# Twelve low-part splits moved behind the last gate, and eight raw loads moved one weight set later

## The reference, cut to what matters

```
attn_out = ...                         # decayed linear attention, 2 x 8 heads x 768 x 64
x = attn_out as 1536 tokens x 512
h = x @ w_in;  g = maximum(0.01 * h, h);  y = g @ w_out       # 512 -> 2048 -> 512
a = y @ w1;  b = y @ w2                                       # 512 -> 1024 each
out = ((a * b) @ w3) @ moe2_w_out                             # 1024 -> 1024 -> 512
```

## Time and profile before

| | us |
|---|---|
| median of 3 runs (519.84 to 519.9) | 519.85 |
| the profiled execution, its own time | 518.86 |
| its span, first to last instruction | 517.0 |
| TensorE busy in it | 507.7 |
| VectorE busy | 354.6 |
| ScalarE busy | 200.7 |

### The profile page before, as it was taken

How to read it: one execution, slowest core, us unless ns; L and a number is a source line. 1 busy time by engine, 2 the same in 40 slices (tenths; PEclk the granted TensorE clock), 3 DMA queues, 4 the chain that set the end, 5 groups by cost and what they waited for, 6 DMA issues and landing times.

```text
span 517.0 us, 9127 instructions
## 1 busy us (share of the span) xinstructions
PE 507.7 (98%) x3580; PEld 418.9 (81%) x3580; DVE 354.6 (69%) x539; ACT 200.7 (39%) x356; POOL 93.8 (18%) x101
## 2 busy tenths in 40 slices
PE   8999999999999999999999999999999999999796
PEld 6788888888888888888888888888888888888585
DVE  4757356767777876687755877697777754799732
ACT  5444253343456533233312455333333315475300
POOL 2223132112102321122200031122333100000000
PEclk9999999999999999999999999999999999999899
DMA  8998582433131111111100212111221107230102
GB/s 292 348 395 296 166 294 85 150 124 125 41 90 39 45 33 42 41 42 41 42 0 1 61 41 83 61 62 61 63 61 62 41 7 279 82 122 0 42 20 102
DMA packets 26666, 51.46 MB, mean 100 GB/s; under 512 B 3824, under 2 KB 4088, under 8 KB 26624
## 3 DMA queue, kind: packets, MB, share of 16 engines
q1 hardware_dynamic: 24144, 43.39, 25.3%
q10 hardware_dynamic: 2448, 7.49, 4.3%
q0 software_dynamic: 32, 0.00, 0.0%
HBM read 45.63 MB, written 5.25 MB: 98 GB/s over the span
## 4 chain that ended last, share of the span: by engine, by line
PE 87%; DVE 7%; DMA 2%; ACT 2%; issue 2%; SPq 1%; DVEq 0%; ACTq 0%
PE acc L1438 11%; PE acc L1439 11%; PE acc L1440 11%; PE hid L1650 10%; PE hid L1651 10%; PE hid L1649 10%; PE hid L1438 5%; PE hid L1440 4%; PE hid L1439 4%; DVE wa_lo L1040 2%; DMA stage<-weights 2%; PE hid L1470 1%; PE hid L1485 1%; PE acc L1777 1%; PE acc L1775 1%
## 5 line engine op out<-in xcount | busy, mean ns | idle before, releaser
L1438 PE MATMUL acc<-g_hi,wb 128*128 128x512 f32 x224 | 87.6, 391 | 0.0
L1440 PE MATMUL acc<-g_hi,wb 128*128 128x512 f32 x224 | 87.2, 389 | 0.0
L1439 PE MATMUL acc<-g_lo,wb 128*128 128x512 f32 x224 | 87.2, 389 | 0.0
L714 POOL TENSOR_TENSOR w_in_lo_place<-stage 128x256 f32<-128x256 f32 x16 | 12.8, 799 | 211.4 <-PE hid L1651 121.0
L1438 PE MATMUL hid<-xy_hi,wa_hi 128*128 128x512 f32 x128 | 50.2, 393 | 0.0
L1440 PE MATMUL hid<-xy_hi,wa_lo 128*128 128x512 f32 x128 | 49.8, 389 | 0.0
L1439 PE MATMUL hid<-xy_lo,wa_hi 128*128 128x512 f32 x128 | 49.8, 389 | 0.0
L1650 PE MATMUL hid<-wa_lo,wa_hi 128*128 128x512 f32 x128 | 49.8, 389 | 0.0
L1651 PE MATMUL hid<-wa_hi,wa_lo 128*128 128x512 f32 x128 | 49.8, 389 | 0.0
L1649 PE MATMUL hid<-wa_hi 128*128 128x512 f32 x128 | 49.8, 389 | 0.0
L1438 PEld LDWEIGHTS acc<-g_hi,wb 128*128 128x128 f32 x224 | 42.0, 188 | 8.9
(11 more groups left out here) (228 smaller groups left out, 935.7 us busy)
## 6 DMA issues: line engine op xcount, KB each, us to landing
stage<-weights SPq DMA_DIRECT2D x109, 256.0 KB, 3.4
w_out_place<-attn ACTq DMA_DIRECT2D x12, 512.0 KB, 5.7
x_hi_place<-attn SPq DMA_DIRECT2D x4, 512.0 KB, 8.5
w_out_place<-attn SPq DMA_DIRECT2D x4, 512.0 KB, 7.4
w_dram<-x_lo_place SPq DMA_DIRECT2D x8, 256.0 KB, 5.4
stage<-w_dram SPq DMA_DIRECT2D x8, 256.0 KB, 2.7
outT<-x_hi_place SPq DMA_DIRECT2D x7, 256.0 KB, 3.0
x_lo_place<-attn SPq DMA_DIRECT2D x2, 512.0 KB, 6.5
```

The source lines that it names most:

```text
L714: nc.gpsimd.tensor_tensor(s_1, a21, a22, ALU.add).then_inc(s_made, 1)
L1438: nc.tensor.matmul(out, w_hi, a_hi, start=first, stop=False)
L1439: nc.tensor.matmul(out, w_hi, a_lo, start=False, stop=False)
L1440: return nc.tensor.matmul(out, w_lo, a_hi, start=False, stop=final)
```

## The change

1. In steps 4 to 7 only the row of T2 is split. T3's four rows are split behind the loop. T4's and B22's eight rows are split two at a time ahead of the four joins of lines 1413 and 1416. The sums themselves are made where they were. ScalarE rounds in the same new order: T3 behind the loop, then the two output copies, then T4 and B22. The counts in `SPLIT_G` follow.
2. SP's eight raw loads stand behind `("again", 5)` instead of `("again", 3)`, so the weights of set 2 are ahead of them in its list.

No instruction is added or taken out on any engine.

```
-SPLIT_G = {name: i for i, name in enumerate([(T1, r) for r in range(ROWS)] +
-                                            [(t, r) for r in range(ROWS) for t in (T2, T3, T4, B22)])}
+SPLIT_G = {name: i for i, name in enumerate([(t, r) for t in (T1, T2, T3, T4, B22) for r in range(ROWS)])}
+SPLIT_AHEAD = [[(T4, 0), (T4, 1)], [(T4, 2), (T4, 3)], [(B22, 0), (B22, 1)], [(B22, 2), (B22, 3)]]
...
-                if ORDER[w] == ("again", 3):
+                if ORDER[w] == ("again", 5):
                     wait_then_step(g1_ready, F2)
                     for f in range(F2):
                         sp.dma_start(raw34(f), w34_dram.ap()[f]).then_inc(raw34_loaded, 16)
...
-                for t in [T1] if f < ROWS else [T2, T3, T4, B22]:
-                    right_hi(t, f % ROWS)
+                right_hi(T1 if f < ROWS else T2, f % ROWS)
+            for row in range(ROWS):
+                right_hi(T3, row)
             for d in range(2):
                 first_complete(d, 2)
                 nc.scalar.copy(place_of_out(d, 1), acc[:, d, :]).then_inc(out_ready, 1)
+            for t in (T4, B22):
+                for row in range(ROWS):
+                    right_hi(t, row)
...
-                for t in [T1] if f < ROWS else [T2, T3, T4, B22]:
-                    right_lo(t, f % ROWS)
+                right_lo(T1 if f < ROWS else T2, f % ROWS)
...
+            for row in range(ROWS):
+                right_lo(T3, row)
             for d in range(2):
+                for name in SPLIT_AHEAD[d]:
+                    right_lo(*name)
                 dve.wait_ge(pair_ready, 2 + d + 1)
                 dve.wait_ge(first_copied, d + 1)
                 nc.vector.tensor_tensor(second_of_out(d), ...)
             for d in range(2):
+                for name in SPLIT_AHEAD[2 + d]:
+                    right_lo(*name)
                 dve.wait_ge(pair_ready, 4 + d + 1)
                 nc.vector.tensor_tensor(third_of_out(d), ...)
```

## The result

The changed kernel takes **513.71 us** (median of 4 runs, 513.54 to 514.19), the kernel before 519.85 (4 runs, 519.63 to 519.90). The ratio is 0.9884 with a 95% interval of 0.9867 to 0.9901: by the ratio 6.0 us faster, 5.1 to 6.9 (the medians themselves are 6.1 apart). The forecast was 514.6 with a range of 514.0 to 516.0.

What follows compares the result with a forecast made beforehand. TensorE, busy 507.7 of 517.0 us, was taken as the bound; removing its late-tile stall and slow restart (5.26 us) takes the profiled execution from 518.86 to 513.60, plus 0.99 to the median: 514.6 us, range 514.0 to 516.0.

Steps and rivals of the forecast that it cites:

- What bounds the kernel: TensorE sets the end; its wait for the last low part of `g1` and the slow restart cost 5.26 us.
- slow restart: TensorE at the lower clock behind its stall, 482.72 to 485.79 us: 1.48 us lost.
- VectorE's chain: VectorE's instructions from gate(6) at 471.60 to the last `g_lo`, done at 478.12 us once splits are moved.
- the margin: The last low part ready 0.8 us before TensorE wants it at 478.94, against 3.8 us late before.
- rival B: A rest of the stall stays because VectorE's chain is longer: 514.8 to 515.8 us, up to 517.3; chance 0.09.
- The cover behind the loop: VectorE's idle time during TensorE's last 120 matmuls hides all twelve moved splits; without it, pairs add 4.8 us, T3 2.4.
- Part two costs and gives nothing: Moving the raw loads behind set 2's weights gains VectorE up to 2.0 us at step 0, hidden by TensorE's pace.
- Rival B's price of a short wait: A short TensorE wait costs its length alone, 0.2 to 1.2 us; a clock fall would add up to 1.48.
- the median of the runs, 0.99 above: The median of the runs was put 0.99 us above the profiled execution's 513.60, giving 514.6 us.
- The sum of 5.26: Stall of 3.78 us plus 1.48 us of lower clock, all taken off the profiled execution's 518.86 us.
- some tenths: Allowance for the tail behind the last matmul and the instruction pitch: 514.0 to 515.2 us around the forecast.

Runs made afterwards that it cites:

- experiment 5: Changed kernel with three more VectorE instructions in step 6 ahead of the last `g_lo`, writing to an unread tile: 514.77 us, ratio 0.9920 to the kernel before.
- experiment 2: Changed kernel with the raw loads put back behind again 3, so only the splits are moved: 513.18 us, ratio 0.9887 to the kernel before.
- experiment 11: Changed kernel with the raw loads back behind again 3, run once more on one chip with the changed kernel: 513.65 us, ratio 0.9884 to the kernel before.
- experiment 3: Kernel before with only the raw loads moved behind again 5: 517.53 us, ratio 0.9965.
- experiment 4: Kernel before with only B22's four splits moved behind the loop, raw loads as before: 516.34 us, ratio 0.9952.
- experiment 7: Kernel before with 15 matmuls of unused result put where TensorE stands still: 518.04 us, ratio 0.9978.
- experiment 1: Kernel before, unchanged, run and profiled again: 519.42 us over 12 runs, 518.11 to 520.66.
- experiment 9: Kernel before, unchanged, profiled a third time: 519.28 us.
- experiment 10: Kernel before, unchanged, profiled a fourth time: 519.03 us.

## Why the prediction was right in its steps and missed in its number

**What bounds the kernel.** Right. The wait of TensorE and its slow restart are gone, and the stretch is shorter by their 5.26 us. One reading was wrong without harm: the earlier trace rows has one slice with an 8, not two.

**VectorE's chain.** Right to a few hundredths. Gate(6) on VectorE was put at 471.60 and stands at 472.31 - 0.70 = 471.61; the last `g_lo` was to end at 478.12 and ends at 478.85 - 0.70 = 478.15; the margin was 0.8 and is 0.80, and experiment 5 used it up. This is the chain on which rival B rested.

**The cover behind the loop.** Right. Join 0 was put at 488.67 and stands there (489.37 - 0.70), behind 2.57 us of idle time where 2.6 were named. The splits fit between the joins, the last pair with nothing to spare.

**Part two costs and gives nothing.** Right in the stretch: experiments 2 and 11. Its times stand as forecast: set 2's loads at 416.40 - 0.70 = 415.70, the raw loads at 424.90. Alone it is worth 1.8 us timed (experiment 3), more than the 0.92 us by which it moves VectorE, because it brings the wait down to 2.7 us and, in the profile, the clock is kept.

**Rival B's price of a short wait.** I took the wait alone, and so it is in the profiles but for 0.1 to 0.2 us: waits of 1.1, 2.1 and 2.7 us kept the full clock, five waits of 3.5 to 4.8 us were followed by a stretch at the lower level. The Trainium skill ("TensorE: Matmul & The Clock Gate", Part 1) has the clock fall to its lower level after an idle stretch of some length. The traces agree, with the eight waits just named. That a slow restart is no fixed price of a wait is shown by the traces of experiments 3, 4 and 5, and by the times too for the 1.1 us of experiment 5.

**What failed: "the median of the runs, 0.99 above" and the range around it.** The sum of 5.26 was subtracted from the profiled execution, and its distance to the median of the runs, 0.99 us, was carried over as if it were a constant of the kernel. It is not. The profiled execution of the kernel before was at the low end of its kind: of four profiles it has the earliest start of the stretch (424.11, the others 424.29 to 424.69) and the cheapest stall (5.26 us, the others 5.34 to 5.78). The changed kernel's profiled execution, 514.19, lies above its three other runs: the distance to the median is -0.48 us where the sum has +0.99. That execution itself was forecast at 513.60 and took 0.6 us more, because its stretch begins 0.70 us later, while the median came 0.9 us below its forecast. So for this pair of executions the stretch was sized right to the hundredth, and the two misses have opposite signs. Two sizes were off:
- *The slow restart.* 1.48 us in the sum; 1.7 us in three of four profiles. With the wait's own scatter (3.63 to 4.06, set by when set 2's weights land) the stretch gains 5.46 on average, 0.2 more than the sum. Experiment 7 took the clock's part away and gained 1.3 us in the stretch and 1.1 timed, with a start 0.2 us later than the average of the kernel before.
- *The scatter of the rest.* I allowed "some tenths" for it and so put the low end at 514.0. The pieces ahead of and behind the stretch vary by 0.7 and 0.8 us in seven profiles, and runs of one kernel on one chip spread by up to 2.5 us. Five comparisons on four occasions gave 5.3 to 6.0 us for the same 5.46. A range from 513.3 would have been honest.

**My first explanation fell too.** That the restart is much longer in most executions (experiment 1's H1) is refuted by experiments 7, 9 and 10: it explains 0.2 us of the 0.8. The granted clock says the same, with 0.993 in only one of the 12 runs of experiment 1. The rest, 519.85 - 5.46 = 514.4 against 513.71, is within the interval of that comparison; that it is scatter is argued from this and not shown. Why the start varies, the loads of the first microseconds or something else, was not tested and stays open. So do what decides when exactly the clock falls around a restart, and whether it fell in the runs at 0.997 of experiments 3 and 4.

## What to carry to other kernels

Where an engine off the main path falls behind step by step, look at what it does in each step that is not wanted until later, and at where it will idle later: twelve instructions moved from the one to the other cost nothing and removed the only stall of the last stage. The place behind a loop is only free up to the idle time that a timeline shows there; here 2.03 us held two splits of 0.6 us each.

A long stall of TensorE can cost more than its length, here 1.5 to 1.7 us more. Shortening it from 3.8 to 2.9 us already saved the slow restart in the profile, and filling it with matmuls of no use made the kernel 1.1 us faster.

A forecast made against one profiled execution inherits that execution's luck. Cut two profiles at a common instruction and compare the stretch between; quote the range with the scatter of what lies outside it.

An engine that is behind can pass a late transfer on: 0.4 us of scatter in one transfer's landing stood in TensorE's stall nearly 50 us later. With a margin, or with the transfer issued earlier, it is gone.

## What the runs showed of the hardware that I had not expected

- After a wait of 3.5 us the clock can fall behind the restart: in experiment 1 the first two starts were 0.34 and 0.27 us apart, and only then 0.43. Full speed came back 4.0 us behind the restart.
- Even with the clock kept, the first interval behind a wait was 0.34 us in place of 0.227 (experiments 3, 4, 5 and 7).
- What lies behind the last matmul's start, two VectorE instructions and the last stores, takes 4.4 us in five and 3.7 us in two of the seven profiles of the table, in both kernels and with the same instructions.
